# Three pairs of PSUM banks for the last tile of the second network, and its store issued by two queues

## The reference

```python
kv_pool = kv.reshape(B, H // r, r, W // r, r, C).mean(axis=(2, 4))
k = v = kv_pool.reshape(B, -1, C) @ w_sr            # 768 keys
a = softmax(q @ k.T / sqrt(C))
x = a @ v
h = x @ moe_w_in                                     # 128 -> 2048
x = (h * sigmoid(1.702 * h)) @ moe_w_out             # 2048 -> 128
h = x @ moe2_w_in                                    # 128 -> 2048
out = (h * clip(h + 3, 0, 6) / 6) @ moe2_w_out       # 2048 -> 128
```

## Time and profile before

| | us |
|---|---|
| median of 3 runs (lowest, highest) | 1311.92 (1311.71, 1314.39) |
| the profiled execution, its whole time | 1314.29 |
| its span, first to last instruction | 1312.6 |
| PE busy | 1277.8 (97%) |
| DVE busy | 1037.8 (79%) |
| ACT busy | 1031.9 (79%) |

### The profile page before, as it was taken

The page is one execution under the profiler, slowest core; times in us unless marked ns, Lnnn a source line. Parts: engine busy times, 40 slices in busy tenths (PEclk is TensorE's granted clock), DMA queues, the critical chain, the costliest instruction groups (busy, mean ns, idle before and its releaser), DMA issues.

```text
span 1312.6 us, 18302 instructions
## 1 busy us (share of the span) xinstructions
PE 1277.8 (97%) x5748; PEld 1061.8 (81%) x5748; DVE 1037.8 (79%) x1073; ACT 1031.9 (79%) x1211; POOL 36.1 (3%) x43
## 2 busy tenths in 40 slices
PE   6799999999999999999999999999999999999996
PEld 6578888888888888888888888888888888888775
DVE  4777788888888888788888887887887788888666
ACT  2678788788888888788888878878888788888665
POOL 1900000000000000000000000000000000000000
PEclk9999999999999999999999999999999999999999
DMA  8332203213023032131130320311302303203000
GB/s 269 91 73 53 64 9 72 48 24 72 22 50 72 0 72 48 24 72 31 41 72 5 67 58 14 72 41 31 72 15 57 66 6 72 48 16 65 9 0 17
DMA packets 186948, 65.94 MB, mean 50 GB/s; under 512 B 108720, under 2 KB 179504, under 8 KB 186672
## 3 DMA queue, kind: packets, MB, share of 16 engines
q1 hardware_dynamic: 186928, 65.69, 22.3%
HBM read 23.13 MB, written 6.34 MB: 22 GB/s over the span
## 4 chain that ended last, share of the span: by engine, by line
PE 94%; DVE 3%; ACT 2%; DMA 1%; issue 0%; SPq 0%; DVEq 0%; ACTq 0%
PE pair L791 16%; PE pair L793 15%; PE pair L792 15%; PE bank_av L791 9%; PE bank_av L792 9%; PE bank_av L793 9%; PE bank_out L791 7%; PE bank_out L792 6%; PE bank_out L793 6%; PE pair L805 1%; DMA kv_sb<-in_kv_dram 1%; DVE mid_lo L665 1%; DVE neg_max L599 0%; DVE work L658 0%; ACT work L446 0%
## 5 line engine op out<-in xcount | busy, mean ns | idle before, releaser
L665 DVE TENSOR_TENSOR mid_lo<-work,mid_hi 128x1024 fp32r<-128x1024 f32 (+1 forms) x193 | 234.9, 1218 | 135.4 <-ACT mid_hi L459 135.2
L791 PE MATMUL pair<-x_hi,w_hi 128*128 128x512 f32 x768 | 302.6, 394 | 6.0 <-DVE x_lo L641 3.7
L792 PE MATMUL pair<-x_lo,w_hi 128*128 128x512 f32 x768 | 299.7, 390 | 0.0
L793 PE MATMUL pair<-x_hi,w_lo 128*128 128x512 f32 x768 | 299.6, 390 | 0.0
L431 ACT ACTIVATE work<-pair 128x1024 f32<-128x1024 f32 x192 | 197.0, 1026 | 127.1 <-PE pair L793 124.9
L649 DVE TENSOR_TENSOR mid_lo<-work,mid_hi 128x1024 fp32r<-128x1024 f32 x192 | 235.8, 1229 | 32.4 <-ACT mid_hi L438 32.4
L658 DVE SCALAR_TENSOR_TENSOR work<-work,pair 128x1024 f32<-128x1024 f32 (+1 forms) x193 | 232.5, 1205 | 10.3 <-ACT work L446 10.2
L446 ACT ACTIVATE work<-pair,half 128x1024 f32<-128x1024 f32 (+1 forms) x193 | 212.1, 1099 | 12.4 <-PE pair L793 11.8
L438 ACT ACTIVATE mid_hi<-work 128x1024 fp32r<-128x1024 f32 x192 | 202.8, 1056 | 5.6 <-PE bank_av L793 3.4
L459 ACT ACTIVATE mid_hi<-work 128x1024 fp32r<-128x1024 f32 (+1 forms) x193 | 201.5, 1044 | 0.5 <-DVE work L658 0.5
L791 PEld LDWEIGHTS pair<-x_hi,w_hi 128*128 128x128 f32 x768 | 144.5, 188 | 44.8 <-ACT work L431 7.1
(11 more groups left out here) (87 smaller groups left out, 1506.3 us busy)
## 6 DMA issues: line engine op xcount, KB each, us to landing
p_keys<-p_turned SPq DMA_DIRECT2D x368, 96.0 KB, 2.2
inv_b<-inv_dram SPq DMA_DIRECT2D x24, 256.0 KB, 3.3
q_raw<-in_q_dram SPq DMA_DIRECT2D x92, 64.0 KB, 2.0
out_dram<-y_sb SPq DMA_DIRECT2D x92, 64.0 KB, 2.4
kv_sb<-in_kv_dram SPq DMA_DIRECT2D x7, 768.0 KB, 11.1
w_raw<-in_moe_w_in_dram SPq DMA_DIRECT2D x2, 1024.0 KB, 8.0
inv_dram<-inv_t SPq DMA_DIRECT2D x96, 0.5 KB
kv_sb<-in_kv_dram SPq DMA_DIRECT2D x3, 256.0 KB, 11.5
```

The costliest lines, as they stand in the source:

```text
L665: dve.tensor_tensor(mid_lo[mid2(t, p)][:, part], act2[p % 2][:, part], mid_hi[mid2(t, p)][:, part], ALU.subtract).then_inc(mid2_ready, 1)
L791: pe.matmul(dst, a_hi, b_hi, start=start, stop=False)
L792: pe.matmul(dst, a_hi, b_lo, start=False, stop=False)
L793: return pe.matmul(dst, a_lo, b_hi, start=False, stop=stop)
```

## The change

PE does h0 ahead of P7' instead of behind it. From h2 on, the last tile uses the bank pair p mod 3 instead of p mod 2, so h2 waits for the first network's last reader of `pair[2]` (`act1_ready`), and h3 and later for the hard_swish three pairs back instead of two. ACT's gate and DVE's hard_swish read the bank pair by the same rule (`hidden2_in`). The last tile is turned in one piece and stored in four DMAs of 64 KB, two issued by SP and two by ACT, instead of eight of 32 KB, all by SP.

```diff
+        def hidden2_in(t, p):
+            return pair[p % 3 if isinstance(t, int) and t == NT - 1 else p % 2]
...
+        def store_columns(queue, t, c):
+            src = y_sb[32 * c:32 * (c + 1), :].rearrange("p (b k) -> p b k", k=32)
+            dst = out_rows[:, bass.ds(t * BLOCKS, BLOCKS), 32 * c:32 * (c + 1)]
+            queue.dma_start(dst, src).then_inc(y_in_dram, 16)
...
-            for part in range(2):
-                store_y(NT - 1, part)
-            sp.wait_ge(y_in_dram, 16 * 4 * (NT + 1))
+            hold(y_ready, NT)
+            for c in range(2):
+                store_columns(sp, NT - 1, c)
+            sp.wait_ge(y_in_dram, 16 * 4 * NT)
...
-                act.activation(gate2[p % 2][:, part], pair[p % 2][:, part], ACT.Relu,
+                act.activation(gate2[p % 2][:, part], hidden2_in(t, p)[:, part], ACT.Relu,
...
+            act.wait_ge(y_ready, NT)
+            for c in (2, 3):
+                store_columns(act, NT - 1, c)
...
-                                         in1=pair[p % 2][:, part], op0=ALU.min,
+                                         in1=hidden2_in(t, p)[:, part], op0=ALU.min,
...
-                dve.transpose(y_sb[:, cols], bank_out[:, cols]).then_inc(y_ready, 1)
+                dve.transpose(y_sb[:, :], bank_out[:, :]).then_inc(y_ready, 1)
...
-            for part in range(2):
-                turn_y(NT - 1, part)
+            turn_y(NT - 1)
...
+                elif isinstance(t, int) and t == NT - 1 and p == 2:
+                    pe.wait_ge(act1_ready, PAIRS * NT)
+                elif isinstance(t, int) and t == NT - 1 and p > 2:
+                    pe.wait_ge(act2_ready, n - 2)
                 elif later(n - 1):
                     pe.wait_ge(act2_ready, n - 1)
-                hidden(pair[p % 2], 2, p, x2_hi, x2_lo).then_inc(h2_ready, 1)
+                hidden(hidden2_in(t, p), 2, p, x2_hi, x2_lo).then_inc(h2_ready, 1)
...
+            hidden2(NT - 1, 0)
             finish_job(NT - 1, JOBS - 1)
+            hidden2(NT - 1, 1)
+            hidden2(NT - 1, 2)
             for p in range(PAIRS):
-                hidden2(NT - 1, p)
-                if p > 1:
-                    project2(NT - 1, p - 2)
-            project2(NT - 1, PAIRS - 2)
-            project2(NT - 1, PAIRS - 1)
+                project2(NT - 1, p)
+                if p + 3 < PAIRS:
+                    hidden2(NT - 1, p + 3)
```

More of the change, by code:

```diff
@@ L223, in of_pair @@
             return slice(0, PAIR) if c is None else slice(c * TILE, (c + 1) * TILE)
-        def of_tile(part):
-            return slice(0, TILE) if part is None else slice(part * TILE // 2, (part + 1) * TILE // 2)
         def later(value):
             return not isinstance(value, int) or value > 0
+        def store_columns(queue, t, c):
+            src = y_sb[32 * c:32 * (c + 1), :].rearrange("p (b k) -> p b k", k=32)
+            dst = out_rows[:, bass.ds(t * BLOCKS, BLOCKS), 32 * c:32 * (c + 1)]
+            queue.dma_start(dst, src).then_inc(y_in_dram, 16)
         block = ctx.enter_context(nc.Block())
@@ L287, in spread_p, with store_y @@
                         sp.dma_start(dst[:, a], src[:, g]).then_inc(p_landed, 16)
-            def store_y(t, part=None):
-                hold(y_ready, t + 1 + (part or 0))
-                cols = of_tile(part)
+            def store_y(t):
+                hold(y_ready, t + 1)
                 for c in range(4):
-                    src = y_sb[32 * c:32 * (c + 1), cols].rearrange("p (b k) -> p b k", k=32)
-                    rows = bass.ds(t * BLOCKS + cols.start // 32, (cols.stop - cols.start) // 32)
-                    sp.dma_start(out_rows[:, rows, 32 * c:32 * (c + 1)], src).then_inc(y_in_dram, 16)
+                    store_columns(sp, t, c)
             def next_q(u):
@@ L666, in act2_lo, with turn_y @@
                                   mid_hi[mid2(t, p)][:, part], ALU.subtract).then_inc(mid2_ready, 1)
-            def turn_y(t, part=None):
-                cols = of_tile(part)
+            def turn_y(t):
                 dve.wait_ge(out2_done, PAIRS * (t + 1))
-                if later(t) and not part:
+                if later(t):
                     dve.wait_ge(y_in_dram, 16 * 4 * t)
-                dve.transpose(y_sb[:, cols], bank_out[:, cols]).then_inc(y_ready, 1)
+                dve.transpose(y_sb[:, :], bank_out[:, :]).then_inc(y_ready, 1)
             for g in range(6):
```

## The result

| | before | the change |
|---|---|---|
| median (lowest, highest) of 22 runs each, same chips | 1312.76 us (1311.2, 1314.95) | 1310.68 us (1308.52, 1313.02) |
| ratio to before, 95% interval | | 0.9983 (0.9976, 0.999) |
| profiled execution: time, span | 1314.29, 1312.6 | 1312.06, 1310.3 |

The change saves 0.17%, 2.2 us (1.3 to 3.2). The forecast took 3.9 us off the median known then, which gave 1308.0 us. The measured time lies in the range, but the saving is little more than half of what was computed. The interval of the ratio does not reach 1, so the saving is real, but it is under the 0.2% that the prediction had set as what can be told from no change. The question is where the rest went.

The account below looks back on a forecast made before the run. The prediction took PE, busy 94% of the span, as the bound, with time won where it waits or after it finishes. 1.91 (hand-over) + 0 (third pair) + 2.0 (store) = 3.9 us off 1311.92 gave 1308.0 us, range 1306.9 to 1311.0.

Parts of the forecast that it names:

- The hand-over: At the start of the last tile, h0 ahead of P7' lets P0 start 1.91 us earlier.
- Three pairs worth nothing: In the last tile's loop no bank is on the path, so a third bank pair gains 0.
- h2's early issue buys nothing: Ahead of P0, h2 goes earlier but PE's next step is still P0, so 0 gained, at most 0.83 us.
- The store: At the end, from the last turn's start to the last landing 3.5 us instead of 5.5, a gain of 2.0.
- rival B: At the last store, both queues act as one: 4.14 us, gain 1.37, total 3.3, 1308.6 us; chance 0.22.
- Rival E: PE's longer wait ahead of P0 lowers its clock once, 1.6 us lost: 2.3 gained, 1309.6 us; chance 0.05.
- The sum: Over the whole tail, 1.91 + 0 + 2.0 = 3.9 us saved, giving a median of 1308.0 us, 0.30% less.
- The chances: For the whole time, faster 0.66, same (within 0.2%) 0.30, slower 0.04.
- Rival F: From P0 to the end the clock stays at 1.2 GHz: 10.8 us slower, 1322.7 us; chance 0.04.

Follow-up runs that it names:

- e2_two_pairs: The change with only two pairs of banks in rotation, h0 ahead of P7' and the two-queue store kept; ratio to before 0.998.
- e4_pairs_only: The change with P7' again ahead of h0, three pairs and the new store kept; ratio to before 0.9998.
- e6_one_queue: The change with all four last DMAs of 64 KB issued by SP; ratio to before 0.998.
- g1_change_again: The change run again with no other edit, beside the filler kernels on one chip; ratio to before 0.9982.
- e1_fill6: The change with six more matmuls, their result unused, between h2 and P0; ratio to before 0.9983.
- the fillers: The change with six or three more matmuls, their result unused, between h2 and P0; their 40 runs average 1309.68 us.

## Why the prediction was right or wrong

**The hand-over** was right, and 0.15 smaller: from x2_lo to P0 10.61 us before, 8.85 now, 1.76 against 1.91. P7' was not delayed by a named wait, but its six matmuls took 1.47 us instead of 1.38, near the 1.51 of a restart; mid_lo ended at 1276.93, only 0.07 ahead of P7'. That this small margin is the reason is likely, not shown. The rest is hundredths at each step behind it. turn_y went out of the way as computed: hard_swish 1 (1281.20) waits for gate 1 and for nothing else.

**Three pairs worth nothing** was right: e2_two_pairs and the change have the same P0 to 0.02 us, and ratios that can't be told apart. But the sentence "h2's early issue buys nothing" left out that it also costs. The wait goes from h2 to behind it, into one wait of 2.24. With h0 ahead this happens with two pairs too (2.22 in e2_two_pairs); without h0 ahead it is the third pair that does it (2.61 in e4_pairs_only).

**The store** was right in kind, and the term was 0.23 too large: 4.18 instead of 3.95 from turn to end, 1.77 gained against 2.0. The landings took up to 2.6 us with two queues at once; I had let all end at 2.7 after the first issue, and they ended at about 3.0. Of this term three quarters came with one queue (the number of DMAs and the single turn), which the prediction had worked out only under rival B. There the sum fits: 4.14 us to the landing, and 0.45 more to the end of the span as before, is 4.59, against 4.61 in e6_one_queue. The Trainium skill ("DMA: Bandwidth & Descriptors", section "Issuing engines are not separate DMA queues") calls what a second issuing engine saves usually small beside the transfer. Here the second queue saved 0.43 of 4.61 us, so that holds better than I granted.

**The clock** is the step that failed: the sum had nothing for it. Rival E named the place, the length of the wait (2.2), the stretch (3.41 us at 0.50) and the price (1.6 us) as they came, and I gave it 0.05. The reason given, that 1.54 us had left the clock alone and 3.28 had not, did not bear so small a chance for a value between the two. The runs put in its place: of five profiled executions with a wait of 2.22 to 2.61 ahead of P0 the clock fell in three, of eight with up to 1.56 there (before included) in none. In the change itself it fell in one execution and not in another. On average this took 1.1 us. How likely a fall is between 1.56 and 2.22 us was not measured.

**The sum** with measured terms: 1.76 + 1.77 - 1.1 = 2.4, against 2.2 (1.3 to 3.2) from the ratio. The terms close within the interval. The median came out at 1310.68, 2.7 above the 1308.0 of the forecast. Of that 0.8 is that before itself had a median of 1312.76 over 22 runs, against 1311.92 over the three shown, and the rest is what the saving fell short. So the range held, with 0.3 to spare, because it was drawn to hold the rivals, and not because its likeliest path came true. Rival E, put on the later median of before, gives 1310.4.

**The chances** were too high for faster. With the measured 1.1 us for the clock the forecast would have been 1309.1. Rival F's price was added up wrongly: from P0 on there are 78 matmuls, three times 24 and 6, and not 18 behind. At the clock it assumed it would have been 8.4 us slower and not 10.8; the forecast doesn't rest on it.

## What to carry to other kernels

Before issuing a step earlier, ask what the engine does behind it. If its next step is held by the same chain, the early step can merge two short waits into a long one. Here a wait of 2.2 us or more was followed, in three traces of five, by 3.41 us at half clock, at a price of about 1.6 us, nearly the 1.76 that the hand-over had won. What helps is one more step of real work between: here h3 ahead of P0 was worth 3.6 us of shorter tail beyond the 1.8 of the hand-over, and two pairs of banks were enough for it. In the short final transfer of this kernel, going from eight DMAs to four was worth 1.34 us, and the second queue 0.43.

## What the runs showed of the hardware that I had not expected

The same program with the same wait of 2.24 us ran its next 3.41 us at 1.2 GHz in one profiled execution and at 2.4 GHz in another. Near the start, where all kernels are the same, PE waits 2.73 to 3.31 us in every trace. In twelve of the thirteen a slow stretch follows or begins inside the wait: 3.41 us in nine, as in before, and 6.8 us in three, here in g1_change_again:

```profile
50.68 0.80 PE L796 MATMUL pair<-x_hi,w_hi 128*128 128x512 f32 x1 [2.73 <-DVE x_lo L648]
```

```profile
49.96:56.78 6.82, 6.10 (x14) 4.79 (x15) 3.40 (x4) 3.54 (x5) 6.27 (x8) 0.50 0.01 2
```

In the thirteenth, e1_fill6, PE also waited 2.73 us and there was none:

```profile
51.17 0.50 PE L796 MATMUL pair<-x_hi,w_hi 128*128 128x512 f32 x1 [2.73 <-DVE x_lo L648]
```

```profile
47.00:56.00 9.00, 5.93 (x24) 4.05 (x23) 6.41 (x10) 6.17 (x9) 8.27 (x9) 1.00 0.01 2
```

So the length of the wait alone does not settle it. What makes the start of x2_lo differ by up to 3.6 us was not looked into further. The clock near the start does not order it: e6_one_queue had a slow stretch there and e1_fill6 none, and they reach x2_lo at 1272.37 and 1272.07; g1_change_again had twice as long a one and reaches it at 1274.09, ahead of before. Single runs of this kernel can't be compared to better than that; pieces of a trace, counted from a common instruction, repeat to about 0.1 us where the clock is the same (29.69 to 29.81 us from x2_lo to the turn with the fillers).
